# A MoE layer on one Trainium2 core: the last tokens of an expert as a half tile of 128

## The reference

```python
# MoE: x [3072, 384], 8 experts, w1 [8, 384, 1024], w2 [8, 1024, 384]
logits = x @ w_gate + modality_bias[modality_id]
e_idx = np.argmax(logits, axis=1)              # one expert per token
...
for e in range(E):
    mask = e_idx == e
    h = np.maximum(x[mask] @ w1[e], 0.0)
    out[mask] = gate_w[mask, None] * (h @ w2[e])
# FFN on the result: [3072, 384] -> 1536 -> 384
rms = np.sqrt(np.mean(x * x, axis=-1, keepdims=True) + 1e-06)
xn = x / rms * rms_g
g = xn @ w_gate
silu = g * (1.0 / (1.0 + np.exp(-g)))
out = (silu * (xn @ w_val)) @ w_out
```

## Time and profile before

| | us |
|---|---|
| median of 3 runs | 845.7 (845.15 to 847.56) |
| the profiled execution | 846.57 |
| its span, first to last instruction | 844.4 |
| TensorE busy in it | 820.2 (97%) |
| VectorE busy | 340.3 (40%) |
| ScalarE busy | 301.6 (36%) |
| mean granted TensorE clock | 0.994 of full |

### The profile page before, as it was taken

One profiled execution on the slowest core, in us unless ns is written; L12 is line 12 of the kernel. 1 busy time (PEld: TensorE's weight loads), 2 busy tenths in 40 slices (PEclk: granted clock), 3 DMA queues, 4 the chain that ended last, 5 costly groups with the idle time before them and its releaser, 6 DMA issues.

```text
span 844.4 us, 14912 instructions
## 1 busy us (share of the span) xinstructions
PE 820.2 (97%) x5277; PEld 747.6 (89%) x5277; DVE 340.3 (40%) x661; ACT 301.6 (36%) x741; POOL 151.2 (18%) x146
## 2 busy tenths in 40 slices
PE   7999996999999999998999999999999999999998
PEld 6888884799999999997889889988988998898888
DVE  6999997632326323233340243034114403521320
ACT  6887883333336333333231222022212302221220
POOL 5988651322112222120000000000000000000000
PEclk9999998999999999999999999999999999999999
DMA  8888742422244222111000100200010010000000
GB/s 261 268 259 255 257 128 94 153 74 86 88 140 147 75 85 93 49 58 42 1 1 29 47 0 11 66 0 0 19 56 0 9 47 19 0 19 19 1 1 37
DMA packets 29035, 63.15 MB, mean 75 GB/s; under 512 B 4787, under 2 KB 17359, under 8 KB 28993
## 3 DMA queue, kind: packets, MB, share of 16 engines
q1 hardware_dynamic: 24224, 52.71, 19.6%
q0 software_dynamic: 3584, 9.46, 3.4%
q10 hardware_dynamic: 1184, 0.45, 0.2%
HBM read 49.62 MB, written 14.56 MB: 76 GB/s over the span
## 4 chain that ended last, share of the span: by engine, by line
PE 82%; DVE 2%; issue 0%; ACT 0%
PE bank L1306 79%; PE bank L1299 1%; PE bank L1349 1%; PE bank L1265 1%; DVE row_hot L1017 1%; DVE col_hot L1014 0%; PE bank L1201 0%; DVE xn_lo L1135 0%; DVE xg_lo L1042 0%; ACT xn_hi L787 0%; DVE place L1004 0%; ACT xg_hi L726 0%; PE bank L1286 0%; ACT o_sb L812 0%; DVE chosen L888 0%
## 5 line engine op out<-in xcount | busy, mean ns | idle before, releaser
L1306 PE MATMUL bank<-xn_hi,ffn_hi 128*128 128x512 f32 x432 | 168.9, 391 | 2.9 <-DVE xn_lo L1135 2.9
L1306 PE MATMUL bank<-xn_hi,ffn_lo 128*128 128x512 f32 x432 | 168.6, 390 | 0.0
L1306 PE MATMUL bank<-xn_lo,ffn_hi 128*128 128x512 f32 x432 | 168.6, 390 | 0.0
L1154 DVE TENSOR_TENSOR prod<-silu,bank 128x512 f32<-128x512 f32 x72 | 49.5, 687 | 281.3 <-ACT silu L800 281.3
L800 ACT ACTIVATE silu<-bank 128x512 f32<-128x512 f32 x72 | 43.1, 598 | 221.1 <-PE bank L1306 221.1
L1306 PEld LDWEIGHTS bank<-xn_hi,ffn_hi 128*128 128x128 f32 x432 | 81.5, 189 | 19.9 <-issue 3.1
L1306 PE MATMUL bank<-ffn_hi,hh 128*128 128x384 f32 x288 | 97.1, 337 | 0.0
L1306 PEld LDWEIGHTS bank<-xn_hi,ffn_lo 128*128 128x128 f32 x432 | 81.4, 188 | 17.0
L1306 PEld LDWEIGHTS bank<-xn_lo,ffn_hi 128*128 128x128 f32 x432 | 81.5, 189 | 16.8
L1306 PE MATMUL bank<-ffn_hi,hl 128*128 128x384 f32 x288 | 96.3, 335 | 0.0
L1306 PE MATMUL bank<-ffn_lo,hh 128*128 128x384 f32 x288 | 96.3, 334 | 0.0
(11 more groups left out here) (164 smaller groups left out, 1284.4 us busy)
## 6 DMA issues: line engine op xcount, KB each, us to landing
rk_in<-rk_t SPq DMA_DIRECT2D x24, 448.0 KB, 4.3
rkn_in<-rk_n SPq DMA_DIRECT2D x24, 384.0 KB, 4.7
ffn_raw<-ffn_w SPq DMA_DIRECT2D x12, 576.0 KB, 3.8
w_raw<-w SPq DMA_DIRECT2D x16, 384.0 KB, 4.3
y_in<-y_tok SPq DMA_DIRECT2D x6, 770.0 KB, 4.5
v_in<-v_n SPq DMA_DIRECT2D x24, 192.0 KB, 4.0
x_tok<-x_sb SPq DMA_DIRECT2D x24, 192.0 KB, 2.3
out<-o_sb SPq DMA_DIRECT2D x24, 192.0 KB, 1.9
```

The lines of the kernel that those rows point to most:

```text
L1154: v.tensor_tensor(prod[f % 2][:], silu[f % 2][:], ps_v[f % 2], ALU.mult).then_inc(prod_ready, 1)
L1306: last = pe.matmul(dst, left[a], right[b2], start=first and n == 0, stop=end and n == 2)
```

## The change

An expert's count is cut differently. It gets whole tiles as long as more than 128 of its tokens are left; what then remains (1 to 128 tokens) is a half. Whole tiles of all experts come first, then the halves. Two halves share one tile of 256 places, with one gather and one scatter, even if they are of different experts. An item is one expert's work on a tile or a half (`ITEMS` of them at most). With 1503 and 1569 tokens this gives 6 and 6 whole tiles and one half (33 tokens of expert 6), which is alone in its tile. Before it was 6 and 7 tiles.

```diff
-NTE = B * S // TE + E - 1
-NG = (NTE + 1) * SUB
+FEW = 8
+MOST = 15
+TILES = 16
+ITEMS = MOST + E + 1
+NG = (TILES + 1) * SUB
...
+PAIRED = FULL - FEW
...
-        def over_tiles(eng, body, n):
-
-            body(0, True)
-            with eng.Fori(1, FULL) as j:
-                body(j, True)
+        def over_tiles(eng, whole_tile, half_tile, no_half, n_whole, n_half):
+
+            whole_tile(0, (0, 1))
+            with eng.Fori(1, PAIRED) as j:
+                whole_tile(j, (2 * j, 2 * j + 1))
+            with eng.Fori(PAIRED, FEW) as j:
+                whole_tile(j, (PAIRED + j,))
 
             def rest(j):
-                with eng.If(j < n):
-                    body(j, False)
-                    if j + 1 < NTE:
+                with eng.If(j < n_whole):
+                    whole_tile(j, ())
+                    if j + 1 < MOST:
                         rest(j + 1)
 
-            rest(FULL)
+            rest(FEW)
+
+            def halves(m):
+                with eng.If(m < n_half):
+                    half_tile(n_whole + m, n_whole + m // 2, 0)
+                    with eng.If(m + 1 < n_half):
+                        half_tile(n_whole + m + 1, n_whole + m // 2, 1)
+                        if m + 2 < E:
+                            halves(m + 2)
+                    with eng.If(n_half < m + 2):
+                        no_half(n_whole + m // 2)
+
+            halves(0)
```

ScalarE, where a tile's result, a half tile and the missing second half are now functions of their own (VectorE has the same shape, its `no_half` is `tile_low(j + 1)`):

```diff
+            def half_tile(i, j, s):
+                hidden(i, slice(s * P, (s + 1) * P), SUB * j + s)
+                if s == SUB - 1:
+                    wait(act, xg_ps, j + 2)
+                    tile_high()
+                next_weights(i)
+                leave_out(j, s)
+
+            def no_half(j):
+
+                wait(act, xg_ps, j + 2)
+                tile_high()
+                wait(act, ye_ready, SUB * j + 1)
+                act.sem_inc(ye_ready, 1)
```

TensorE:

```diff
+            def tile(j, pieces):
+                up(j, j, slice(0, TE))
                 turn_tile(j + 1)
...
+                for s in range(SUB):
+                    down(j, j, s, s == 0)
+
+            def half_tile(i, j, s):
+                up(i, j, slice(s * P, (s + 1) * P))
+                if s == SUB - 1:
+                    turn_tile(j + 1)
+                down(i, j, s, True)
+
+            over_tiles(pe, tile, half_tile, lambda j: turn_tile(j + 1), n_whole, n_half)
```

VectorE's sorting chain (the operations before `order`, then those after it):

```diff
-            then(v.tensor_reduce(tiles[:], over[:], AX_X, ALU.add))
-            then(v.tensor_tensor_scan(tiles_upto[:], ones_b[:, 0:E], tiles[:], 0.0, ALU.mult, ALU.add))
-            v.tensor_scalar(none[:], tiles_upto[:], 0.0, None, ALU.is_le)
+            then(v.tensor_reduce(whole[:], over[:], AX_X, ALU.add))
+            v.tensor_tensor_scan(upto_e[:, 0, :], ones_b[:, 0:E], whole[:], 0.0, ALU.mult, ALU.add)
+            then(v.scalar_tensor_tensor(rest_n[:], whole[:], -float(TE), count[:], ALU.mult, ALU.add))
+            v.tensor_scalar(half[:], rest_n[:], 0.0, None, ALU.is_gt)
+            v.tensor_scalar(none[:], upto_e[:, 0, :], 0.0, None, ALU.is_le)
...
+            v.scalar_tensor_tensor(limit[:], whole[:], float(TE), before[:, :, 0], ALU.mult, ALU.add)
-            then(v.tensor_tensor(start[:], tiles_upto[:], tiles[:], ALU.subtract))
+            then(v.tensor_tensor(start[:], upto_e[:, 0, :], whole[:], ALU.subtract))
+            v.tensor_tensor_scan(half_upto[:], ones_b[:, 0:E], half[:], 0.0, ALU.mult, ALU.add)
             v.tensor_reduce(expert_f[:], none[:], AX_X, ALU.add)
+            v.tensor_tensor(in_half[:], place_e[:], limit[:].unsqueeze(2).to_broadcast([P, E, NT]), ALU.is_ge)
...
+            v.tensor_tensor(half_start[:], half_upto[:], half[:], ALU.subtract)
+            v.tensor_scalar(half_shift[:], upto_e[:, 0, :], upto_e[:, 0, E - 1:E], -float(TE), ALU.subtract, ALU.mult)
             then(v.tensor_tensor(place_e[:], place_e[:], shift[:].unsqueeze(2).to_broadcast([P, E, NT]), ALU.add))
+            then(v.scalar_tensor_tensor(half_shift[:], half_start[:], float(P), half_shift[:], ALU.mult, ALU.add))
+            then(v.tensor_tensor(in_half[:], in_half[:], half_shift[:].unsqueeze(2).to_broadcast([P, E, NT]), ALU.mult))
+            then(v.tensor_tensor(place_e[:], place_e[:], in_half[:], ALU.add))
...
+            v.tensor_scalar(pair[:], iota[:, 0:E:2], n_half_f, None, ALU.is_lt)
+            then(v.tensor_scalar(upto_e[:, 1, :], half_upto[:], n_whole_f, None, ALU.add))
+            v.tensor_reduce(pairs[:], pair[:], AX_X, ALU.add)
+            then(v.tensor_tensor(done[:], upto_e[:].rearrange("p a e -> p (a e)").unsqueeze(1).to_broadcast([P, ITEMS, 2 * E]),
+                                 iota[:, 0:ITEMS].unsqueeze(2).to_broadcast([P, ITEMS, 2 * E]), ALU.is_le))
+            v.tensor_copy(tile_counts[:, 0:1], n_whole_f)
+            v.tensor_copy(tile_counts[:, 1:2], n_half_f)
+            v.tensor_tensor(tile_counts[:, 2:3], pairs[:], n_whole_f, ALU.add)
...
+            then(v.tensor_scalar(wrap[:], done_n[:], float(E), float(E), ALU.is_ge, ALU.mult))
+            then(v.tensor_tensor(expert_n[:], done_n[:], wrap[:], ALU.subtract))
```

More of the change, by code:

```diff
@@ L138, in build @@
         over = sb("over", [P, E, FULL], F32, logits)
-        tiles = sb("tiles", [P, E], F32, logits)
-        tiles_upto = sb("tiles_upto", [P, E], F32, logits)
+        whole = sb("whole", [P, E], F32, logits)
+        rest_n = sb("rest_n", [P, E], F32, logits)
+        half = sb("half", [P, E], F32, logits)
+        upto_e = sb("upto_e", [P, 2, E], F32, logits)
+        half_upto = sb("half_upto", [P, E], F32, logits)
         none = sb("none", [P, E], F32, logits)
         expert_f = sb("expert_f", [P, 1], F32, logits)
-        done = sb("done", [P, NTE + 1, E], F32, logits)
-        done_n = sb("done_n", [P, NTE + 1], F32, logits)
-        moved = sb("moved", [P, NTE + 1], F32, logits)
+        done = sb("done", [P, ITEMS, 2 * E], F32, logits)
+        done_n = sb("done_n", [P, ITEMS], F32, logits)
+        wrap = sb("wrap", [P, ITEMS], F32, logits)
+        expert_n = sb("expert_n", [P, ITEMS], F32, logits)
+        moved = sb("moved", [P, ITEMS], F32, logits)
+        pair = sb("pair", [P, E // 2], F32, logits)
+        pairs = sb("pairs", [P, 1], F32, logits)
         start = sb("start", [P, E], F32, logits)
         shift = sb("shift", [P, E], F32, logits)
+        limit = sb("limit", [P, E], F32, logits)
+        half_start = sb("half_start", [P, E], F32, logits)
+        half_shift = sb("half_shift", [P, E], F32, logits)
+        in_half = sb("in_half", [P, E, NT], F32, logits)
         place_e = sb("place_e", [P, E, NT], F32, logits)
@@ L765, in tile @@
+            def tile(j, pieces):
+                hidden(j, slice(0, TE), SUB * j)
                 wait(act, xg_ps, j + 2)
                 tile_high()
[L768 to L773, removed]
@@ new lines, in tile @@
+            def tile(j, pieces):
+                hidden(j, j, 0, slice(0, TE))
+                tile_low(j + 1)
+                next_weights(j)
+                for n in pieces:
+                    wait(dve, fw_hi, n + 1)
+                    v.tensor_tensor(ffn_lo[:, bass.ds(n, 1), :], ffn_raw[:].unsqueeze(1),
+                                    ffn_hi[:, bass.ds(n, 1), :].bitcast(F32), ALU.subtract).then_inc(fw_lo, 1)
+            def half_tile(i, j, s):
+                hidden(i, j, s, slice(s * P, (s + 1) * P))
+                if s == SUB - 1:
+                    tile_low(j + 1)
+                next_weights(i)
@@ L1102, in means @@
+            over_tiles(dve, tile, half_tile, lambda j: tile_low(j + 1), n_whole, n_half)
             def means(i):
@@ L1321, in tile, with down @@
                                 wait(pe, xg_split, 2 * j + 2)
[L1322 to L1323 removed]
+                            last = product(ps_h[q][:, f, toks], (w1_hi[:, q, k, cols], w1_lo[:, q, k, cols]),
+                                           (xg_hi[:, k, toks], xg_lo[:, k, toks]), k == 0, k == KD - 1)
                     last.then_inc(h_ps, 1)
+            def down(i, j, s, first):
+                toks = slice(s * P, (s + 1) * P)
+                wait(pe, ye_ready, SUB * j)
+                for f in range(FC):
+                    q = f // FPQ
+                    if first and f % FPQ == 0:
+                        wait(pe, w_split, 2 * EQ * i + EQ + q + 1)
+                        wait(pe, h_split, EQ * i + q + 1)
+                    last = product(ps_ye[s], (h_hi[:, f, toks], h_lo[:, f, toks]),
+                                   (w2_hi[:, q, f % FPQ, :], w2_lo[:, q, f % FPQ, :]), f == 0, f == FC - 1)
+                last.then_inc(ye_ps, 1)
+            def tile(j, pieces):
+                up(j, j, slice(0, TE))
                 turn_tile(j + 1)
```

147 lines of the change are left out of this document (74 added, 73 removed).

## The result

| | us |
|---|---|
| before, median of 5 runs | 847.47 (845.15 to 847.56) |
| after, median of 5 runs | 852.15 (849.91 to 854.89) |
| ratio after / before, 95% interval | 1.0064 (1.0037 to 1.0091) |
| profiled execution, before / after | 846.57 / 849.91 |
| its span | 844.4 / 848.1 |

The changed kernel is slower by 0.64%. The forecast was 849.6 against 845.7, a ratio of 1.0046, and slower.

A forecast was written before the change was run, and what follows sets the result against it. TensorE was taken to bound the kernel. Tile 12 with the way out +2.1, sorting before `order` +1.6 and behind it +0.2 gave +3.9 us: 850.5 on the profiled execution, 849.6 as median, range 845.5 to 853.

The forecast's parts named there:

- What bounds: TensorE, busy 820.2 of 844.4 us, alone is the chain from the first tile, except before it and before the FFN.
- Term 1: Output products of tile 12: one half, 24 matmuls, goes, taking 4.17 us from TensorE's path; 4.17 us stay.
- term 2: Hidden products of tile 12: 72 matmuls of 128 columns at 0.111 us, 8.0 us in all, saving 0.6 us.
- Rival A: Half products go by columns, weight loads hidden: 4.8 us instead of 8.0, time 846.4; chance 0.17.
- rival C: fp32r of 128 columns runs at a quarter of the rate: 8.3 us more, 857.9; chance 0.09.
- Term 3: Way into the FFN after D, the end of tile 12's output products: 12.2 us against 4.64 before, turning coming late.
- Rival B: ScalarE's jump before `tile_high` costs nothing: D + 1.1 instead of D + 2.9, time 847.8; chance 0.12.
- Tile 12 and way out together: From tile 12's start to the FFN: 24.4 us against 22.27 before, a term of +2.1 us.
- Term 4: Sorting chain before `order`, all exposed: 1.75 us of added operations, 0.15 less in `col_hot`, +1.6 us.
- Term 5: Behind `order`: about 1.7 us more before `w_lo`, barely covered by a 2.02 us wait; taken as +0.2 us.
- Edits at nothing: FFN weights in two pieces, GpSimd's last scatter and TensorE's own jumps were taken to cost nothing.
- Rival D: Full saving arrives, FFN preparation as covered as before: 5.5 us less, plus 1.8 of sorting, 842.0; chance 0.04.

The follow-up runs named there:

- short kernel: Changed kernel with the code for whole tiles 12 to 14 and halves 2 to 7, which never runs, left out: 848.22, ratio 1.0014 to the kernel before.

## Why the prediction was right, step by step

**What bounds** held: TensorE alone is the chain from tile 0 on, and nearly all differences lie where it was to be entered or left. The exception is the 0.80 us ahead of tile 12.

**Term 1**, 24 output products, and **term 2**, 72 hidden products at 0.111 us: 8.0 us forecast, 8.04 measured. Rival A (columns decide) falls, by 64 and 192 columns at the same distance; rival C (a quarter of the rate) falls too. That the load, and not some other fixed part of these products, makes the 0.111 is the best reading left, and not shown. By the Trainium skill ("TensorE: Matmul & The Clock Gate", LDWEIGHTS) a load takes 107 ns, and the trace agrees within 5 ns; the figure of some 81 ns for 128 columns (Back-to-back issue gap) doesn't hold for these products.

**Term 3**, the way into the FFN: 12.2 forecast, 12.21 measured. Its parts: `tile_high` at D + 2.9, measured 3.07; from there to `mean` 1.65 + 0.2, measured 1.57, because `mean` starts with the end of `xg_lo` and not 0.2 behind it; `mean` to the last scaling 5.32, measured 5.34; from there to the FFN 2.1, measured 2.23. So errors of 0.1 to 0.3 us cancel in the 12.21. Rival B (no jump) is true only without the code that isn't run. It is also mispriced: D + 1.1 takes TensorE's turning to start at once, but it started 1.26 us late, so that without ScalarE's jump alone some D + 2.1 was left. I took ScalarE's jump for the obstacle that it is; I did not see TensorE's beside it, nor that VectorE has one of 2.8 us, which becomes the bound as soon as the turning is gone. Tile 12 and way out together: 24.4 forecast, 24.71 measured.

**Term 4**: 1.75 us of added operations, measured 1.77, and 0.15 less in `col_hot`, measured 1.23 to 1.08. `row_hot` also shrank, 5.50 to 5.26, which I had at nothing. Net +1.3 instead of +1.6. **Term 5**: `order` to the first product took 8.65 before and 8.67 after, 0.0 where I took 0.2. But the cover was gone, and a little more: `w_lo` started 2.14 us later behind `order` than before (1.7 forecast, against 2.02 of cover), and `xg_lo` started 0.79 us behind `xg_hi` instead of 0.63. The 0.16 don't show, because the transposes came 0.13 earlier behind `order`.

**Edits at nothing**: tiles 1 to 11 kept 17.63 us each, with two pieces of FFN weights or one. But one sentence here failed: "TensorE's own jumps lie under its queue". Ahead of tile 12 TensorE stood 0.80 us (1.11 in the second profile), and ahead of its late turning 1.26. The first is the way over code for further whole tiles into the halves, since the short kernels don't have it. It is TensorE's own jump and not VectorE's, to which my expectation for the short kernel gave it: VectorE's signal for kept weights (L1153) comes 0.03 us behind TensorE's last output product, so VectorE stood ready there, and all that TensorE needs for tile 12's first products stands before this signal in VectorE's program. The 0.74 us begin only behind it.

**What the sum lacked**: the granted clock. It took 1.46 us in tile 0 and gave 1.24 back in the FFN's first block; with the 0.80 and the 1.0 that the attention was shorter, the profiled execution came out at 3.3 above its counterpart where I forecast 3.9. That these two are so close is luck: +0.80, +1.46, −1.24 and −1.02 were in no term and nearly cancel. The fair comparison is the change's own part, 4.56 us, against 3.9: 0.80 came on top, tile 12 and the way out cost 0.34 more than forecast, and the sorting 0.5 less. The medians, 4.7 and 4.2 us apart in two comparisons, lie on both sides of 4.56. The clock falling in tile 12 now and then may stand behind runs of up to 854.9; that is argued and not shown. Rival D (the full saving arrives, 842.0, which is 3.7 us under the kernel before) fell for the changed kernel for the reason given, VectorE's program order, and for a second one, VectorE's jump. With the turning and the unused code gone, the kernel came near it, 3.1 us under the kernel before; what is missing is mostly the cover that a tile of half the length can't give.

## What to carry to other kernels

Work on the bounding engine is also the cover of everything beside it: before a tile is shortened, list what the other engines do under it, in their program order, and price it from the tile's new end (here 5.1 us saved, 7.6 lost). Code for cases that don't occur isn't free where a program jumps over it with nothing queued: it cost TensorE 0.8 and 1.3 us, ScalarE 1.9 and VectorE 2.8 here, and the next such jump hides under the one found first. These fp32r products, each with its own 128-column load, gain 0.009 us each when the moving side goes from 256 columns to 192, and nothing below.

## What the runs showed of the hardware

- An fp32r matmul with a new 128-column weight load costs 0.111 us at 64, 128 and 192 moving columns and 0.120 at 256.
- A wait named "issue" on the way out of nested branches was 1.7 to 2.1 us on ScalarE, 2.7 to 2.8 on VectorE, and on TensorE 1.3 to 1.5 in four of seven profiles and less in the other three. With the unused code gone it was 0, 0.5 and 0. The Trainium skill ("Runtime: NRT & Kernel Launch", Instruction fetch mechanics) says that a branch to code outside the fetched pages stalls; the runs agree in that the waits went with the code between, and that the instruction queues then carried 4 packets there instead of 16.
- The granted clock can fall to 0.50 after TensorE has been busy without a gap for 2.4 or 4.0 us, behind a hole of 0.9 or 1.1 us: 2 of 11 profiles, 6.4 us each. It isn't only narrow products: in tile 0 of the repeated changed kernel and of the 192-column one, the first products of 256 columns ran at 1.00 and the fall came 0.6 and 0.8 us into them.
- At tile 0 the granted clock differs between executions of the same code. In the changed kernel the fillers ended at 152.18, and the first product came 3.24 us later, at 0.50; in the kernel before it came 2.37 us later, at 1.00. The other three profiles with some 10.4 us for tile 0's hidden products had 2.8 us or more there, the other nine with 8.90 had 2.1 to 2.6. The 14 filler instructions took 5.8 us in two of the profiles with a slow tile 0, and 6.1 to 7.4 in all others with 7 fillers. When the fillers end relative to the gather seems to decide; the three profiles with 8 or 10 fillers fit it and don't prove it.
